# A fused attention and two feed-forward kernel: keys times values moved from the end of a unit to the start of the next window

## What is computed

```python
f = 1.0 / (1.0 + np.exp(-f_logit))
for t in range(S):
    state = f[:, :, t, :, None] * state + np.einsum('bhd,bhe->bhde', k[:, :, t], v[:, :, t])
    y[:, :, t] = np.einsum('bhd,bhde->bhe', q[:, :, t], state)
...
h = x @ w_in                                   # 3072 x 384 times 384 x 2048
g = where(h >= 1, h, where(h <= -1, 0, (h + 1) ** 2 / 4))
x = g @ w_out
...
g = x @ w_gate                                 # 384 x 1536
out = (silu(g) * (x @ w_val)) @ w_out2
```

## Time and profile before

| | us |
|---|---|
| median of 3 runs | 1028.82 (1027.88 to 1028.92) |
| the profiled execution | 1029.0 |
| its span, first to last instruction | 1027.2 |
| PE busy in the span | 994.6 (97%) |
| DVE, ACT, POOL busy | 489.2, 466.1, 427.3 |
| first feed-forward layer starts (first `hidden`) | 57.1 |

### The profile page before, as it was taken

The page is one execution under the profiler, slowest core; times in us unless marked ns, Lnnn a source line. Parts: engine busy times, 40 slices in busy tenths (PEclk is TensorE's granted clock), DMA queues, the critical chain, the costliest instruction groups (busy, mean ns, idle before and its releaser), DMA issues.

```text
span 1027.2 us, 19928 instructions
## 1 busy us (share of the span) xinstructions
PE 994.6 (97%) x8277; PEld 828.3 (81%) x8277; DVE 489.2 (48%) x615; ACT 466.1 (45%) x851; POOL 427.3 (42%) x360
## 2 busy tenths in 40 slices
PE   4789999999999999999999999999999999999998
PEld 4668688888888888888888888888888888888886
DVE  7879948745954874584355422222222222232221
ACT  5865667657667765766355322221222222221221
POOL 6759736652763665385265222222222222222222
PEclk9999999999999999999999999999999999999999
DMA  9540133015005201300541010010100100000000
GB/s 353 197 157 2 63 108 151 1 45 184 32 3 173 86 2 51 116 32 2 185 139 47 1 62 1 10 53 1 58 4 1 62 1 1 32 0 1 31 1 32
DMA packets 17802, 63.61 MB, mean 62 GB/s; under 512 B 1968, under 2 KB 2352, under 8 KB 16944
## 3 DMA queue, kind: packets, MB, share of 16 engines
q1 hardware_dynamic: 17712, 62.33, 16.8%
HBM read 52.89 MB, written 9.44 MB: 61 GB/s over the span
## 4 chain that ended last, share of the span: by engine, by line
PE 89%; POOL 4%; issue 2%; DVE 2%; ACT 1%; DMA 1%; SPq 0%; ACTq 0%; POOLq 0%; DVEq 0%
PE acc L568 11%; PE acc L569 10%; PE acc L570 10%; PE bank L595 7%; PE bank L594 7%; PE bank L596 7%; PE hid L554 6%; PE hid L556 6%; PE hid L555 6%; PE bank L407 4%; PE hid L595 2%; PE hid L594 2%; PE hid L596 2%; POOL keys L1117 2%; PE bank L474 2%
## 5 line engine op out<-in xcount | busy, mean ns | idle before, releaser
L1159 POOL TENSOR_TENSOR g_lo<-prod,g_hi 128x512 fp32r<-128x512 f32 x72 | 93.1, 1293 | 347.7 <-ACT g_hi L846 347.7
L1152 POOL TENSOR_TENSOR g_lo<-act_tmp,g_hi 128x512 fp32r<-128x512 f32 x96 | 127.3, 1326 | 166.2 <-ACT g_hi L807 166.2
L1050 DVE TENSOR_TENSOR sig<-sig,bank 128x512 f32<-128x512 f32 x72 | 49.5, 688 | 275.4 <-ACT sig L840 275.4
L846 ACT CAST g_hi<-prod 128x512 fp32r<-128x512 f32 x72 | 44.7, 621 | 248.1 <-PE acc L570 248.1
L1117 POOL TENSOR_TENSOR keys<-keys,gates 128x512 f32<-128x512 f32 x82 | 107.9, 1317 | 73.3 <-PE bank L407 48.3
L554 PE MATMUL hid<-x_hi,win_hi 128*128 128x512 f32 (+1 forms) x291 | 117.0, 402 | 2.8 <-DVE act_tmp L1038 2.4
L568 PE MATMUL acc<-g_hi,wout_hi 128*128 128x512 f32 x288 | 114.2, 397 | 1.2 <-POOL g_lo L1152 1.2
L556 PE MATMUL hid<-x_hi,win_lo 128*128 128x512 f32 (+1 forms) x291 | 113.7, 391 | 0.0
L555 PE MATMUL hid<-x_lo,win_hi 128*128 128x512 f32 (+1 forms) x291 | 113.4, 390 | 0.0
L569 PE MATMUL acc<-g_lo,wout_hi 128*128 128x512 f32 x288 | 112.3, 390 | 0.0
L570 PE MATMUL acc<-g_hi,wout_lo 128*128 128x512 f32 x288 | 112.2, 390 | 0.0
(11 more groups left out here) (102 smaller groups left out, 1932.9 us busy)
## 6 DMA issues: line engine op xcount, KB each, us to landing
gates<-in_f_dram SPq DMA_DIRECT2D x12, 512.0 KB, 5.1
queries<-in_q_dram SPq DMA_DIRECT2D x12, 512.0 KB, 4.9
keys<-in_k_dram SPq DMA_DIRECT2D x12, 512.0 KB, 4.7
values<-in_v_tok_dram SPq DMA_DIRECT2D x6, 1024.0 KB, 7.5
q_tok<-in_q_tok_dram SPq DMA_DIRECT2D x12, 384.0 KB, 7.7
k_tok<-in_k_tok_dram SPq DMA_DIRECT2D x12, 384.0 KB, 8.2
x_dram<-x_out SPq DMA_DIRECT2D x6, 768.0 KB, 3.3
x_raw<-x_dram SPq DMA_DIRECT2D x6, 768.0 KB, 5.5
```

The lines of the kernel that those rows point to most:

```text
L1152: pool.tensor_tensor(g_lo[:, c % RING, :], act_tmp[:, 2 + c % 2, :], g_hi[:, c % RING, :].bitcast(F32), ALU.subtract).then_inc(g_lo_done, 1)
```

## The change

Keys times values go to visit HS + 6 for unit 0 and HS + 2 for units 1 to 4, which are the visits in which the next unit's level one stands, and in front of it. The add goes one visit behind that, and for unit 0 `place_state` moves by four visits too. `keys_tok` of units 1 to 4 now lies on `q_tok` and the start of `k_tok`; ACT's first copy into it waits until the next unit's use of these is over, and the token copies of the unit after that are loaded when keys times values have read it. Gates are loaded in front of keys, once the unit before has done its last scaling and the decay of the state.

```diff
-             kv=HS + 2, state=HS + 3, state_place=HS + 5)
+             kv=HS + 6, state=HS + 7, state_place=HS + 9)
...
-             tk=y + 2, tk_out=(y + 3, y + 3, y + 4), kv=y + 4, state=y + 5, state_place=HS + 5)
+             tk=y + 2, tk_out=(y + 3, y + 3, y + 4), kv=HS + 2, state=HS + 3, state_place=HS + 5)
...
+    tok = place
     q_tok = att("q_tok", [P, B * DM])
...
-    keys_tok = [at(n, o, [P, BP * 2 * D + R - D]) for n, o in (("keys_tok0", X + 2 * KC * UT * 4), ("keys_tok", A))]
+    keys_tok = [at(n, o, [P, BP * 2 * D + R - D]) for n, o in (("keys_tok0", X + 2 * KC * UT * 4), ("keys_tok", tok))]
...
             elif a > 1:
-                sp.wait_ge(filled, fill(a, 0))
+                sp.wait_ge(q_scaled, scaled(a - 1, SCALES))
+                sp.wait_ge(k_scaled, a * SCALES)
+                sp.wait_ge(g_merged, merges(a, 0))
+                sp.wait_ge(state_decayed, a - 1)
...
         def load_tok(a, gs=(0, 1)):
             if a > 0:
                 sp.wait_ge(diag_done, 2 * a)
+            if a > 2:
+                sp.wait_ge(filled, fill(a - 1, 0))
...
             load_q(a)
-            if a == 1:
-                load_f(a)
+            load_f(a)
             load_k(a)
-            if a > 1:
-                load_f(a)
             load_v(a)
...
         def take_last_keys(a):
             act.wait_ge(x_lo_done, (a + 1) * B)
             if a > 0:
-                act.wait_ge(state_decayed, a)
+                act.wait_ge(diag_done, 2 * (a + 2))
```

## The result

| | before | with the change |
|---|---|---|
| median of 8 runs | 1028.87 us (1027.45 to 1030.11) | 1031.3 us (1030.56 to 1033.04) |
| ratio | | 1.0028, 95% interval 1.0018 to 1.0039 |
| profiled execution, span | 1027.2 | 1028.8 |

What follows compares the result with a forecast made beforehand. PE was taken to bound the kernel, busy 994.6 of 1027.2 us. Terms 2.00 + 1.8 - 0.6 = +3.2 us, set against the median of 1028.8, gave 1032.0 us; range 1029.4 to 1034.0.

Steps and rivals of the forecast that it cites:

- Unit 0: First window: the group leaves a PE wait for DVE, gaining 0, and costs 2.00 us at visit 6.
- Unit 1: Of 2.8 us freed in the first window 0.2 arrive; the group costs 2.00 in the second: +1.8 us.
- Units 2 to 4: Each group leaves a place costing 2.20 us for one costing 2.00: -0.2 each, -0.6 us.
- from one small group to the other: PE's step between keys times values and level one: bounds 0 and 0.2 us, taken as 0.
- The add and the loads: Level one's second group waits for DVE's add with 1.3 us to spare; moved loads are not waited for: 0.
- The clock: PE's half-clock stretch from 69.0 to 72.4 us, costing some 1.7 us, is in both kernels: no change.
- Two stretches of half clock: Rival: PE's longer first-window wait brings half clock sooner and for two stretches, up to +1.7 us, 1033.7; chance 0.12.
- the first window swallows: Rival: waits between 97 and 122 us absorb unit 0's 2.00 us, leaving +1.2 us, 1030.0; chance 0.08.

Runs made afterwards that it cites:

- spread placings: The changed kernel with two of unit 2's four placings of the diagonal one visit later; 1030.02 us, ratio 1.0016 to the kernel before.
- loads alone: The changed kernel with all groups at their old visits, keeping only keys_tok's new place, the gates' earlier load and the waits with it; 1028.60 us.
- both back: The changed kernel with unit 0's and unit 1's groups back in their old visits; 1027.66 us, ratio 0.9991 to the kernel before.
- the two kernels with 8 matmuls: The changed kernel with unit 0's group back and 8 unit-matrix matmuls behind it: 1028.87 us; the same with spread placings: 1027.61 us.
- the fillings: Unit-matrix matmuls in PE's wait: changed kernel with 34, 1032.10 us, 16, 1030.41; spread placings, unit 0 back, 16, 1028.59; and the two kernels with 8 matmuls.

## Why the prediction was right

Forecast 1032.0, measured 1031.3, slower as forecast, by 2.4 us between the medians and 2.5 in the trace where 3.2 were forecast.

**Unit 0: +2.0 forecast, +1.89 measured.** The wait of 4.3 us came as 4.09. The reading that decided it, that a group inside a wait is free, is shown by putting it back. So is the other, that all that follows hangs on level one's fill: DVE's takes start 1.86 us later behind chunk 2 (10.99 against 9.13), and the rest of the window keeps its length. It holds in executions with half clock behind the wait, as said below.

**Unit 1: +1.8 forecast, +1.77 measured** (1.87 in the second window less 0.10 in the first). The three waits came as 0.33, 0.26 and 1.24 us where 0.4, 0.6 and 1.4 were forecast. Relative to ACT's rows project 13 starts 0.25 us earlier than before (157.51 - 0.88 = 156.63 against 156.88), 0.2 forecast; 0.1 of it arrives at the second window. The spread placings show the cause.

**Units 2 to 4: -0.6 forecast, -1.04 measured.** The mechanism was right and the size off. The step is the one "from one small group to the other", for which I took 0: it is below 0. A group next to level one costs 1.87, not the 2.00 of its stay between large ones, since the records of the group and of level one overlap at their seam: level one starts 1.90 us behind the group's start. With all five groups priced 0.13 us lower the forecast would have been 0.65 us lower, nearly all of the 0.7 by which it is too high. I kept bounds for that step from 0 up, with no end below.

**The add and the loads: 0 forecast, 0 measured.** DVE is 1.2 us early for the bank (1.3 forecast), and loads alone give a ratio of 0.9999 (0.9990 to 1.0007) and windows of the old length.

**The clock: no change forecast.** In the profiled pair there is none, 3.4 us of half clock each. But the two further mechanisms I kept as rivals both exist in part. Two stretches of half clock were seen once, 0.9 us, in a kernel with the longer wait. And where no half clock falls, the first window swallows 0.8 us of unit 0's group, since DVE and the ACT copy that it waits for, and not PE, are then what is late. This rival had 0.08. That the forecast for unit 0 came out so close is in part luck: it was read from an execution with half clock, and the execution profiled after had it too. I had read DVE's wait of 0.23 us in front of its takes as a sign that DVE is not the pace. That held in an execution in which PE had just lost 1.6 us to its clock (eight steps of 0.427 us instead of 0.23): in "both back" and in the two kernels with 8 matmuls, which have unit 0's group in its old visit and met no half clock there, the wait is gone, and the takes start 2.5 us behind PE's level one instead of 1.2. The Trainium skill (TensorE: Matmul & The Clock Gate, under Why this matters for your kernels) warns of long idle gaps of PE. The runs bear this out only in part: idle time of 2.17 us was followed by half clock, 3.05 us in "both back" was not, and whether the fillings kept the full clock is not shown. What they do show is that, from chunk 2 on, the full clock is worth only 0.3 to 1.1 us of the 1.6, depending on who is late next.

## What to carry to other kernels

Work of the bounding engine that lies inside one of its waits is free, and taking it out gives nothing; look for the release that ends the wait and ask whether it depends on the work. Where a large hole opens instead, follow the feeding engines through it, chunk by chunk: here ACT's gapless 6 us let 0.1 of 2.7 us through. Find the point on which the rest of a stage hangs and time up to it and behind it apart: here that was one take of DVE, with 81.2 to 81.35 us behind it in nine kernels. And a slack read from one execution may belong to a stretch of half clock just before it, so ask what is late when the clock holds.

## What was not expected of the hardware

- A matmul of a 128 x 128 float32 unit matrix by itself takes 0.22 us on PE (34 in 7.5), in two records 0.112 us apart; a transpose of the same size in the same kernel is one record and takes 0.10 us (15 in 1.55).
- Two groups of small matmuls with 64 columns of weights overlap at their seam: 1.90 us from start to start and 4.08 for the pair, against 2.00 and 2.21 for each alone between large ones.
- POOL's subtraction of 128 x 512 took 2.06 us in place of 1.29 while DVE's product of 128 x 1024 ran beside it, and that product took 3.44 for two in place of 2.35 at unit 3. In the change's own trace, at the same two products, it was 2.07 and 3.45. That each slows the other is read from their overlap; it was not tried.
